# Two DMA loads outstanding instead of three at the head of a fused attention and mixture-of-experts kernel, and one VectorE operation moved ahead of two others

## Time and profile before

| | us |
|---|---|
| three executions | 507.1, 507.39, 511.4 |
| median | 507.39 |
| the profiled execution | 507.1 |
| its span on the core | 505.4 |
| TensorE busy, of the span | 488.9 |
| VectorE, ScalarE, GpSimd busy | 310.7, 219.4, 163.0 |

### The profile page before, as it was taken

One profiled execution on the slowest core, in us unless ns is written; L12 is line 12 of the kernel. 1 busy time (PEld: TensorE's weight loads), 2 busy tenths in 40 slices (PEclk: granted clock), 3 DMA queues, 4 the chain that ended last, 5 costly groups with the idle time before them and its releaser, 6 DMA issues.

```text
span 505.4 us, 9481 instructions
## 1 busy us (share of the span) xinstructions
PE 488.9 (97%) x3531; PEld 403.6 (80%) x3531; DVE 310.7 (61%) x677; ACT 219.4 (43%) x384; POOL 163.0 (32%) x190
## 2 busy tenths in 40 slices
PE   7899999999999999999999999999999999999992
PEld 4788888888888887888888778898888888888882
DVE  4576565454257775325777787855578878638760
ACT  3654545443231122113211556324367858847620
POOL 2411010000000000300000037164157999999942
PEclk9999999999999999999999999999999999999998
DMA  8899731498500000201233336125796978956000
GB/s 261 278 293 260 244 87 44 132 324 256 166 1 1 0 2 0 85 0 43 84 90 115 91 140 191 44 85 150 233 362 213 334 304 303 339 201 250 24 28 33
DMA packets 26719, 76.93 MB, mean 152 GB/s; under 512 B 5279, under 2 KB 5279, under 8 KB 26400
## 3 DMA queue, kind: packets, MB, share of 16 engines
q1 hardware_dynamic: 22656, 69.77, 42.4%
q0 software_dynamic: 4000, 6.32, 3.5%
HBM read 62.92 MB, written 19.96 MB: 164 GB/s over the span
## 4 chain that ended last, share of the span: by engine, by line
PE 88%; DVE 3%; issue 3%; ACT 3%; DMA 2%; POOL 0%; ACTq 0%; POOLq 0%; DVEq 0%
PE bank L1361 10%; PE bank L1362 10%; PE bank L1363 10%; PE bank L1405 8%; PE bank L1407 8%; PE bank L1406 8%; PE bank L1374 7%; PE bank L1638 3%; PE bank L1376 3%; PE bank L1640 3%; PE bank L1641 3%; PE bank L1642 3%; PE bank L1352 2%; DMA tile_in<-attention_tiles 2%; PE bank L1498 2%
## 5 line engine op out<-in xcount | busy, mean ns | idle before, releaser
L391 POOL TENSOR_TENSOR w_lo<-raw,w_hi 128x256 fp32r<-128x256 f32 x104 | 91.7, 915 | 11.0 <-ACT w_hi L375 11.0
L666 ACT ACTIVATE g<-bank 128x512 f32<-128x512 f32 x48 | 28.6, 596 | 134.4 <-PE bank L1363 134.2
L579 POOL DMA_INDIRECT dispatched_rows<-rows,slot_idx x12 | 12.8, 1071 | 219.4 <-DVE slot_idx L1074 216.6
L375 ACT ACTIVATE w_hi<-raw 128x1024 fp32r<-128x1024 f32 x80 | 82.0, 1049 | 0.2 <-issue 0.2
L391 DVE TENSOR_TENSOR w_lo<-raw,w_hi 128x1024 fp32r<-128x1024 f32 (+1 forms) x60 | 70.1, 1179 | 18.8 <-ACT w_hi L375 18.7
L1361 PE MATMUL bank<-x_hi,w_hi 128*128 128x512 f32 x192 | 77.1, 402 | 0.4 <-DVE x_lo L936 0.4
L1405 PE MATMUL bank<-w_hi,g_hi 128*128 128x512 f32 x192 | 77.2, 402 | 0.0
L1407 PE MATMUL bank<-w_hi,g_lo 128*128 128x512 f32 x192 | 75.8, 395 | 0.0
L1406 PE MATMUL bank<-w_lo,g_hi 128*128 128x512 f32 x192 | 75.8, 395 | 0.0
L1362 PE MATMUL bank<-x_lo,w_hi 128*128 128x512 f32 x192 | 75.7, 394 | 0.0
L1363 PE MATMUL bank<-x_hi,w_lo 128*128 128x512 f32 x192 | 75.6, 394 | 0.0
(11 more groups left out here) (154 smaller groups left out, 817.8 us busy)
## 6 DMA issues: line engine op xcount, KB each, us to landing
raw<-expert_units SPq DMA_DIRECT2D x64, 512.0 KB, 6.3
raw<-dense_units SPq DMA_DIRECT2D x16, 512.0 KB, 4.7
tile_in<-attention_tiles SPq DMA_DIRECT2D x12, 592.0 KB, 5.5
dispatched_rows<-empty SPq DMA_DIRECT2D x26, 257.0 KB, 8.0
slot_rows<-dispatched_rows SPq DMA_DIRECT2D x26, 257.0 KB, 3.2
tile_in<-attention_tiles SPq DMA_DIRECT2D x12, 384.0 KB, 6.3
gate_rows<-gate_rows SPq DMA_DIRECT2D x2, 1024.0 KB, 5.2
out<-rows,e_token POOLq DMA_INDIRECT x16, 3.7
```

The lines of the kernel that those rows point to most:

```text
L375: act.activation(w_hi[u % RING][:, :], raw[u % RING][:, :], ACT.Copy).then_inc(s_whi, 1)
L391: last = engine.tensor_tensor(w_lo[u % RING][:, part], raw[u % RING][:, part], w_hi[u % RING][:, part].bitcast(F32), ALU.subtract)
```

## The change

SyncE's list keeps the order of its transfers, and every wait stands one transfer earlier: two are issued at the start, and each later one is issued when the second last before it has landed. VectorE's steps 1 to 8 do `x_low(t)` ahead of `maximum(t + 2)` and `less_max(t + 2)` instead of behind them. Nothing is added or removed besides one wait at the end of the loop.

```diff
             load_queries_keys(0)
             load_queries_keys(1)
+            landed_queries_keys(0)
             load_queries_keys(2)
-            landed_queries_keys(0)
+            landed_queries_keys(1)
             load_queries_keys(3)
-            landed_queries_keys(1)
+            landed_queries_keys(2)
             load_values(0)
-            landed_queries_keys(2)
+            landed_queries_keys(3)
             load_values(1)
-            landed_queries_keys(3)
+            landed_values(0)
             load_unit(0)
-            landed_values(0)
+            landed_values(1)
             load_values(2)
-            landed_values(1)
+            landed_unit(0)
             load_values(3)
-            landed_unit(0)
+            landed_values(2)
             load_queries_keys(FIRST)
-            landed_values(2)
+            landed_values(3)
             load_unit(1)
-            landed_values(3)
+            landed_queries_keys(FIRST)
             load_queries_keys(FIRST + 1)
-            landed_queries_keys(FIRST)
+            landed_unit(1)
             unit = 2
             for t in range(FIRST, NT):
                 load_unit(unit)
-                landed_unit(unit - 1)
-                load_values(t)
                 if t + 1 < NT:
                     landed_queries_keys(t + 1)
+                load_values(t)
+                landed_unit(unit)
                 if t + 2 < NT:
                     load_queries_keys(t + 2)
-                landed_unit(unit)
+                landed_values(t)
                 unit += 1
...
-                if FIRST <= t < NT - 1:
-                    inverse(t + 1)
+                if FIRST <= t < NT:
+                    if t + 1 < NT:
+                        inverse(t + 1)
+                    x_low(t)
                 if FIRST + 1 < t + 2 < NT:
                     maximum(t + 2, 0)
                     less_max(t + 2, 0)
-                if FIRST <= t < NT:
-                    x_low(t)
```

## The result

The changed kernel takes 511.88 us (median of 20 runs, 510.54 to 513.67), the kernel before 507.95 (median of 20, 505.73 to 511.43): a ratio of 1.0073, 95% interval 1.0053 to 1.0091. The forecast was 507.9 with a range up to 510.0, and no change. It is 0.7% slower, within the 1% that was given as the bound of what can be told, but clear of this measurement's interval and outside the range.

The account below looks back on a forecast made before the run. TensorE, busy 97% of the span, was taken as the bound, with loads mattering only at the start. Loads +0.4, fetch -0.2, VectorE order +0.3 made +0.5 on 507.1, 507.6; as median 507.9 us, range 506.5 to 510.0.

Parts of the forecast that it names:

- L: Time from a load's issue to landing with two outstanding: taken as 4.1 us, ends 3.5 and 4.4; cost 0.4 us.
- The ladder: Loads at the start, each issued when the second last before has landed; QK5 lands at 6.1 + 5 L, 26.6.
- The cover: At scores(2), 0.75 us late by QK2: TensorE reaches the pause at 12.2, before its end at 12.51, which swallows the lateness.
- the pause: TensorE's 1.05 us stop at 11.46 in scores(3), read as being out of instructions until a 16 KB fetch is in.
- The fetch: Instruction fetch ending TensorE's stop in scores(3), perhaps sooner with fewer loads beside it: gain 0.2 us, bounds -0.5 and +0.3.
- The VectorE term: x_low ahead of maximum and less_max delays transposes in steps 1 and 6, by 0.24 and 0.07: cost 0.3 us, ends 0 and 0.7.
- the list of needs: Times by which TensorE or ScalarE needs each load, up to QK5 at 26.91; later loads were said never to be late.
- The base: Starting time of the forecast: the profiled execution's 507.1 us, with the median of three runs 0.3 above it.
- B: Rival: late loads at the start, 4.4 to 4.5 us to landing, QK5 or QK4 holds TensorE; 509.4 us, chance 0.20.
- C: Rival: time to landing stays near 6 us whatever the depth, scores(5) 9.2 us late; about 517.5 us, chance 0.05.
- A: Rival: a gain, shorter stop in scores(3), landing in 3.7 us, edge wait hidden behind x_low; 506.9 us, chance 0.15.
- The case of slower by over 1%: Whole kernel slower by over 1%, about 5 us, through a landing time that stays near 6 us; chance 0.05.

Follow-up runs that it names:

- experiment 7: One load outstanding throughout SyncE's list, against the kernel before: 544.67 us, one run.
- experiments 8 and 10: 8: the kernel before profiled again, 510.39 us. 10: the kernel before with U0's high part split later, 507.40 us, ratio 0.9983.
- experiment 2: Only VectorE's new order, x_low(t) ahead of maximum and less_max, loads as in the kernel before: 510.01 us, ratio 1.0026.
- experiment 1: Only the changed SyncE list of loads, VectorE's order as in the kernel before: 511.83 us, ratio 1.0080.
- experiment 9: The full changed kernel run and profiled once more: 511.73 us.
- experiments 4 and 5: Against the kernel before, 4: three outstanding up to V3, then two, 508.04 us; 5: two up to V0, then three, 509.38 us.

## Why the prediction was wrong

**The step that failed is L, the time to landing with two outstanding.** The prediction said: "If the engines were the limit, two outstanding would give L = 2 x 2.03 = 4.1 ... I take L = 4.1, with 3.5 and 4.4 as the ends." It was 5.0 (4.9 again). Its own formula then gives QK5 at 6.1 + 5 x 4.96 = 30.9; it landed at 30.57, 3.7 us behind the 26.91 at which it had been needed, and TensorE was 3.9 late. The ladder, its links and their needs were right, the rung's length wasn't; and the rungs weren't alike, 2.4 of the 3.9 us over 5 x 4.1 lying in QK3's. Both ends of a better estimate stood in the rows: 3.5 to 3.9 us alone and about 6.1 with three outstanding. Halfway between is 4.9. I scaled the 6.1 by two thirds as if all of it were queueing, though by the table of experiment 7 some 2.5 us of it don't shrink with the queue. QK1 of that experiment, alone from 4.53 to 8.21 us, shows where a load's time beside its bytes goes: 0.9 us from issue to the first packet, half a microsecond in which the first packets bring only 103 GB/s, and 0.3 us from the last packet's end to landing:

```profile
4.53:5.45 0.92, 0.92 (x37) 0.86 (x40) 0.00 (x0) 0.00 (x0) 0.00 (x0) 1.00 0.00 0
5.45:6.00 0.55, 0.55 (x40) 0.42 (x32) 0.26 (x2) 0.00 (x0) 0.00 (x0) 1.00 0.84 103
6.00:7.90 1.90, 0.03 (x4) 0.00 (x0) 1.43 (x4) 0.79 (x2) 0.00 (x0) 1.00 0.73 289
7.90:8.21 0.31, 0.00 (x0) 0.00 (x0) 0.00 (x0) 0.06 (x1) 0.00 (x0) 1.00 0.00 0
```

In the changed kernel the engines idle in the same way. From 17 to 18 us their share is 0.09, little more than one of 16, while V1 (landing at 17.57) and U0 (18.64) are outstanding and what V1 releases has no packet before 18.5:

```profile
17.00:18.00 1.00, 0.38 (x12) 0.39 (x14) 0.84 (x2) 0.02 (x1) 0.00 (x0) 1.00 0.09 37
```

The 4.4 us in the earlier trace rows was taken as an upper end, but that V tile had one neighbour for part of its way and was the smallest transfer. From the share of 0.96 the prediction read that the engines were the limit; over 1 to 28 us it was 0.89, and with four outstanding it rose to 0.96 and the rate from 282 to 308 GB/s, so they weren't full.

The Trainium skill's page "DMA: Bandwidth & Descriptors" gives in its section "Anatomy of one DMA" a fixed part of about 2.0 us plus the bytes at 436 GB/s. The trace agrees in form: alone, 592, 512 and 384 KB took 3.7, 3.4 and 3.3 us. The mean transfer of this list, 509 KB, took 3.7 us alone (3.5 without the two that met an instruction packet), against 3.2 as an estimate by the page. I had used it as a bound for two outstanding that overlap perfectly (1.7 us each), and set it aside for "loads in a crowd", where a part that doesn't shrink with the queue was what counted.

**The cover held, and was worth less.** scores(2) came at 8.78 where 8.6 was said, and values(0) at 13.65 where 13.2 to 13.5 was: the pause had room for the late QK2. But QK3 landed at 12.58 and not 10.2, so the load stood in the pause's place. QK3 took 6.1 to 7.5 us with the list of three and 5.8 to 7.0 with two. Why this one load is slow at either depth is open. An instruction packet may be part of it: alone, such a packet went with about 1.2 us more (experiment 7). In every profile of two outstanding one lies on QK3's way (8.9 to 9.8 us in the changed kernel). With three, QK3 took 6.3, 7.4 and 7.5 us with one on its way, and 6.1 and 6.2 in the two profiles (experiments 8 and 10) in which it came behind the landing. No run moved it by itself.

**The fetch.** The pause went, as the gain of 0.2 assumed, but nothing was gained by it, since QK3 landed behind it: in four profiles with two outstanding no pause named issue stands in the first 28 us. With three, 1.05, 2.95 and 2.98 us in all in three profiles of that list, and 0 and 0.9 in two where QK3 came late; with four and five 2.9 and 2.5. That the pauses are waits for instructions is borne out by the nine ends 1.3 to 1.6 us behind the packets. That the fetch comes late because it queues behind the loads is argued and not shown: no run changed the loads beside it and nothing else. The Trainium skill's page "Runtime: NRT & Kernel Launch", section "Instruction fetch mechanics", calls the crossing of a block mostly hidden. Up to 2.98 us of TensorE's time in one such pause don't agree with that here.

**The VectorE term** of 0.3 was right in experiment 2: 0.33, in the two steps named. **A need was missing:** U2 and U3 weren't in the list of needs, because from scores(5) on the loads were said to gain 2.6 us per tile and "are never late again". They do gain, but from a deficit; U3 was 0.3 us late for split_hi(3), and together with the edge it cost TensorE 0.6 us at tile 5 in the first profile (0.9 in experiment 1, where U3 was 1.0 late, and 0.2 in experiment 9, where it was in time).

**The base.** The profiled execution of before had a short pause. The median of 20 is 0.85 us above it, not 0.3. So the profiled executions differ by 4.9 us and the medians by 3.9: 3.9 from the loads at scores(5), 0.6 at tile 5, 0.2 at tile 10, 0.2 later, less the luck of that profile.

**The rivals.** B had the mechanism and stopped at L = 4.5; at 5.0 its own rule gives QK5 at 31.1, 4.2 late, against the 3.9 measured. C, a landing time that doesn't depend on depth, is excluded: 3.7, 5.0, 6.1, 7.3. A had its shorter pause and lost it to the loads. The case of slower by over 1% didn't come, at 0.7%.

## What to carry to other kernels

In this kernel, up to four outstanding, the time to landing was a part that stays plus n times a transfer's own share: read it alone and at the present depth and interpolate, and don't scale it. Where a list of loads is a ladder (each issued when an earlier one has landed), multiply the error by the number of rungs up to the tightest need, and list every need, those behind the critical stretch too. More outstanding isn't free either: here four made the loads sooner and the kernel 0.3% slower. Of the depths tried, the three of before was faster than two and four, and than one in a single run; five had one run and is not told apart.

## What the runs showed of the hardware

- With one to five loads of 509 KB on average outstanding, one landed every 3.70, 2.48, 2.03, 1.82 and 1.80 us, which makes an estimated 3.7, 5.0, 6.1, 7.3 and 9.0 us to landing; bytes per busy microsecond of the DMA engines stayed at 301 to 328 GB/s.
- Alone, the two loads among whose packets a 16 KB instruction packet fell took 4.9 and 4.3 us, where the others of their sizes took 3.7 to 3.8 and 3.1 to 3.4.
- TensorE stops in the middle of a block of matmuls with nothing to wait for that the profile shows. In scores(3) it is behind the same instruction in all five profiles that have it, for 1.05 to 2.98 us; four more, of 0.34 to 1.75 us, stand in transposes(2) and scores(4). All nine end 1.3 to 1.6 us behind a 16 KB packet on the instruction queue. The start of the kernel before spreads over 3 us by such stops, by the half clock behind them and, in experiment 2, by late loads.
- In both profiles of the changed kernel the granted clock fell to half (1.2 GHz) between 18 and 19 us, after TensorE had idled 1.5, 1.1 and 1.8 us (1.3, 1.2 and 2.0), and came back between 25 and 26; there eight transposes took 1.94 instead of 1.08 us. With the same loads it fell at 13.6 us in experiment 1, after 0.6 and 2.1 us of idling, and with dummy matmuls at 21.5. With the loads of before it fell at 15.05 behind the pause of 2.61 us. It kept its level through the start in the first profile of before and in experiments 4 and 5, of which 5 had idled 1.0, 1.7 and 1.3 us, so these rows give no rule for when it falls.
